# A chunked linear-attention and two-layer MLP kernel: the first group's order is rewritten (twelve idle transposes, output pieces back to back, one state decay on GpSimd, new orders of loads and weight halves)

## The reference, cut to what matters

```python
def _attn_ref(r, k, v, w, u):            # B, H, S, D = 4, 8, 768, 48
    for t in range(S):
        kt, vt, rt, wt = (k[:, :, t], v[:, :, t], r[:, :, t], w[:, :, t])
        cur = np.einsum('bhd,bhe->bhde', u[None] * kt, vt)
        y[:, :, t] = np.einsum('bhd,bhde->bhe', rt, state + cur)
        state = wt[:, :, :, None] * state + np.einsum('bhd,bhe->bhde', kt, vt)
# x: the 3072 tokens x 384 of y
h = x @ w_in                             # 384 -> 2048
g = np.where(h >= 1, h, np.where(h <= -1, 0.0, (h + 1) ** 2 / 4.0))
x = g @ w_out                            # 2048 -> 384
g = x @ w_gate                           # 384 -> 1536
out = ((g / (1 + np.exp(-g))) * (x @ w_val)) @ w_out2
```

## Time and profile before

| | |
|---|---|
| median of 3 runs | 984.63 us (984.63 to 985.52) |
| the profiled execution | 988.26 us, its span 986.4 us |
| PE busy | 961.5 us of the span (97%), mean granted clock 0.996 |
| DVE, ACT, POOL busy | 520.4, 404.3, 149.6 us |

### The profile page before, as it was taken

How to read it: one execution, slowest core, us unless ns; L and a number is a source line. 1 busy time by engine, 2 the same in 40 slices (tenths; PEclk the granted TensorE clock), 3 DMA queues, 4 the chain that set the end, 5 groups by cost and what they waited for, 6 DMA issues and landing times.

```text
span 986.4 us, 17455 instructions
## 1 busy us (share of the span) xinstructions
PE 961.5 (97%) x6874; PEld 942.9 (96%) x6874; DVE 520.4 (53%) x913; ACT 404.3 (41%) x849; POOL 149.6 (15%) x146
## 2 busy tenths in 40 slices
PE   5898999999999999999999999999999999999998
PEld 4788999999999999999999999999999999999997
DVE  7795757666566675675434443434334334434332
ACT  5755546445454554554575322222222222222222
POOL 6582120210202103020253400000000000000000
PEclk9998999999999999999999999999999999999999
DMA  8816131312212122200332201010100101010000
GB/s 244 275 44 165 58 96 44 96 56 74 83 57 80 61 86 58 82 26 1 113 105 85 85 1 49 1 49 1 49 0 0 48 0 48 0 48 0 24 1 26
DMA packets 23493, 59.52 MB, mean 60 GB/s; under 512 B 2689, under 2 KB 12033, under 8 KB 23425
## 3 DMA queue, kind: packets, MB, share of 16 engines
q1 hardware_dynamic: 23424, 58.59, 18.8%
HBM read 49.14 MB, written 9.44 MB: 59 GB/s over the span
## 4 chain that ended last, share of the span: by engine, by line
PE 91%; DVE 3%; DMA 2%; issue 1%; ACT 1%; SPq 0%; POOL 0%; DVEq 0%; ACTq 0%
PE bank L1168 48%; PE bank L1196 34%; PE bank L1222 3%; PE bank L1244 2%; PE bank L1239 2%; PE bank L1250 1%; PE bank L1214 1%; PE bank L1231 1%; DMA r_k_v_by_token<-in_rkv_token 1%; DMA ring<-in_w_gate 1%; DVE glo L1019 1%; DVE gate L1026 0%; DVE suf L929 0%; DVE state_decayed L980 0%; DMA ring<-in_w_out 0%
## 5 line engine op out<-in xcount | busy, mean ns | idle before, releaser
L770 ACT ACTIVATE ghi<-gate 128x384 fp32r<-128x384 f32 x224 | 117.2, 523 | 190.6 <-DVE gate L1038 95.4
L1019 DVE TENSOR_TENSOR glo<-gate,ghi 128x384 fp32r<-128x384 f32 x224 | 133.0, 594 | 114.8 <-ACT ghi L770 112.4
L1036 DVE TENSOR_TENSOR gate<-bank,gate 128x384 f32<-128x384 f32 x96 | 53.5, 558 | 215.0 <-ACT gate L889 215.0
L1168 PE MATMUL bank<-xhi,w2gv_ahi 128*128 128x384 f32 x480 | 161.3, 336 | 0.0
L1168 PE MATMUL bank<-xlo,w2gv_ahi 128*128 128x384 f32 x480 | 161.3, 336 | 0.0
L1168 PE MATMUL bank<-xhi,w2gv_alo 128*128 128x384 f32 x480 | 161.3, 336 | 0.0
L889 ACT ACTIVATE gate<-bank 128x384 f32<-128x384 f32 x96 | 47.2, 492 | 227.7 <-PE bank L1168 227.7
L1196 PE MATMUL bank<-ghi,w1ohi 128*128 128x384 f32 x384 | 134.5, 350 | 0.7 <-DVE glo L1019 0.7
L1168 PE MATMUL bank<-xhi,w1ihi 128*128 128x384 f32 x384 | 129.5, 337 | 5.0 <-DVE gate L1026 2.3
L1196 PE MATMUL bank<-glo,w1ohi 128*128 128x384 f32 x384 | 129.7, 338 | 0.0
L1196 PE MATMUL bank<-ghi,w1olo 128*128 128x384 f32 x384 | 129.6, 337 | 0.0
(11 more groups left out here) (93 smaller groups left out, 1532.0 us busy)
## 6 DMA issues: line engine op xcount, KB each, us to landing
r_k_v_by_token<-in_rkv_token SPq DMA_DIRECT2D x24, 576.0 KB, 5.3
k_r_by_channel<-in_kr_channel SPq DMA_DIRECT2D x24, 448.0 KB, 4.1
w_by_channel<-in_w_channel SPq DMA_DIRECT2D x24, 226.2 KB, 2.7
x_t<-ring SPq DMA_DIRECT2D x8, 576.0 KB, 3.0
x_raw<-x_t SPq DMA_DIRECT2D x8, 576.0 KB, 4.0
ring<-in_w_out SPq DMA_DIRECT2D x22, 192.0 KB, 3.4
out_t<-ring SPq DMA_DIRECT2D x7, 576.0 KB, 3.1
ring<-in_w_gate SPq DMA_DIRECT2D x12, 192.0 KB, 2.3
```

The costliest lines, as they stand in the source:

```text
L770: e.activation(ghi[j % 2][:, :], gate[j % 2][:, :], ACT.Copy).then_inc(M["hi", ph], 1)
L1019: e.tensor_tensor(glo[j % 2][:, :], gate[j % 2][:, :], ghi[j % 2][:, :].bitcast(F32), ALU.subtract)\
L1036: e.tensor_tensor(q, hid[j % 2][:, 0:T], q, ALU.mult).then_inc(M["t", 2], 1)
L1168: m = e.matmul(out, w_of(a, k), x_of(b_, k), start=start and i == 0, stop=stop and i == total - 1)
```

## The change

Only group 0 and what is prepared in it for the groups 1 and 2 is touched. Sizes, tiles and the arithmetic of each instruction stay.

- PE: twelve transposes of the identity into the bank of `KT(2)`, in front of the wait of `KT(2)` for its scaled input. In `FIRST_FILLS` the three `Y` come together, then the three `XT`, then `ST(2)`. Group 1's attention pieces come one slot later (4, 6, 7, 9, 10, 12, 13), and in slot 13 ACT and DVE drain `XT(2)` before their knee.
- The decay of the state for window 2 of group 0 is taken from ACT (8 instructions of 48x48) to POOL (2 of 48x192).
- `lo` halves: DVE keeps chunk 3 alone; POOL makes the other 31. `hi` halves on ACT: 8 in front of the `XT` drains, 9, then 11 behind the first two knees, and then by `HI_FIRST`.
- DVE in front of slot 0: drains of `Y`, then `XT`, then `ST(2)`; `w1_lo(3)`, `suffix_scan(1,0)`, the two knees, and only then `prefix_scan(1,0)` and `sum_w(0)`. Scans, scalings and sums of group 1 move by up to one slot; group 2's scans from slots 10, 13, 14 to 11, 14, 15. `w_beyond` has two halves, so that a check doesn't wait for the sum before.
- SP: the first 13 chunks all come right behind group 0's loads; group 1's loads are mixed with two sets of four chunks; the last chunks come before `load_w(2, w)`.

```diff
                ("KT", 2, 0), ("ST", 1, 0), ("AT", 2, 0), ("AT", 2, 1),
-               ("Y", 1, 0), ("XT", 0, 0), ("Y", 2, 0), ("XT", 1, 0), ("ST", 2, 0), ("XT", 2, 0)]
+               ("Y", 1, 0), ("Y", 2, 0), ("XT", 0, 0), ("XT", 1, 0), ("XT", 2, 0), ("ST", 2, 0)]
+WARM = 12
 NBANK = 3
...
 DIAG_SLOTS = {2: 0, 4: 1, 7: 2}
-WIN_SLOTS = {j: tuple(FILLS.index(f) for f in visit) for j, visit in zip((3, 5, 6, 8, 9, 11, 12), VISITS)}
+def visits_at(slots):
+    return {j: tuple(FILLS.index(f) for f in visit) for j, visit in zip(slots, VISITS)}
+WIN_SLOTS = visits_at((3, 5, 6, 8, 9, 11, 12))
+WIN_FIRST = visits_at((4, 6, 7, 9, 10, 12, 13))
+XT_FIRST = 13
...
-CHECK_FIRST = {0: 1, 2: 2}
-SCAN_FIRST = {1: 1, 4: 2}
-SCALE_FIRST = {0: 0, 2: 1, 7: 2}
-DIAG_FIRST = {2: 0, 4: 1, 6: 2}
-DVE_LO = 4
-LO_FIRST = {0: 7, 1: 11, 3: 15, 4: 19, 6: 23, 8: 27, 10: 31}
-PRODUCTS_AT = {8: 0, 13: 1, 20: 2}
-VALUES_AT = {12: 0, 18: 1, 25: 2}
+CHECK_FIRST = {0: 1, 3: 2}
+SCAN_FIRST = {1: 1, 5: 2}
+SCALE_FIRST = {0: 0, 2: 1, 8: 2}
+DIAG_FIRST = {2: 0, 5: 1, 7: 2}
+SCAN_SLOTS_FIRST = {11: 0, 14: 1, 15: 2}
+DVE_CHUNK = 3
+HI_FIRST = {0: 13, 1: 13, 2: 15, 3: 18, 4: 21, 5: 24, 6: 27, 7: 30, 8: 32}
+PRODUCTS_AT = {10: 0, 17: 1, 22: 2}
+VALUES_AT = {16: 0, 23: 1, 28: 2}
...
+def win_slots(g):
+    return WIN_FIRST if first(g) else WIN_SLOTS
+def scan_slots(g):
+    return SCAN_SLOTS_FIRST if first(g) else SCAN_SLOTS
...
         checked, _ = place("w_checked", [PR, NPAIR * WIN], mybir.dt.bfloat16)
-        beyond, _ = place("w_beyond", [PR, OPS_CHECK], F32)
+        beyond, _ = place("w_beyond", [PR, 2, OPS_CHECK + 2], F32)
         bad, _ = place("w_bad", [PR, OPS_CHECK + 1], F32)
...
         w1_at = at[0]
+        assert w1_at % 64 == 32
         w1i = [place(f"w1i{n}", [P, J1, KT * P], F32R)[0] for n in ("hi", "lo")]
...
-            if (c + 1) % DVE_LO == 0:
-                wait(wlo_d, (c + 1) // DVE_LO)
+            if c == DVE_CHUNK:
+                wait(wlo_d, 1)
             else:
-                wait(wlo, c + 1 - (c + 1) // DVE_LO)
+                wait(wlo, c + 1 if c < DVE_CHUNK else c)
...
             load_tok(0, 2)
-            load_w1(3)
-            for w in range(NW):
-                load_w(1, w)
-            load_w1(RING - 4)
-            for w in range(NW):
-                load_kr(1, w)
-                load_tok(1, w)
-            load_w1(14)
+            load_w1(RING - 1)
+            load_w(1, 0)
+            load_kr(1, 0)
+            load_w(1, 1)
+            load_tok(1, 0)
+            load_w1(4)
+            load_kr(1, 1)
+            load_w(1, 2)
+            load_tok(1, 1)
+            load_w1(4)
+            load_kr(1, 2)
+            load_tok(1, 2)
+            load_w1(2 * J1)
             for w in range(NW):
                 load_w(2, w)
-            load_w1(2 * J1)
...
             def w1_lo(c):
-                if (c + 1) % DVE_LO == 0:
+                if c == DVE_CHUNK:
                     return
...
+            def decay_second():
+                w = 2
+                e.wait_ge(scan, OPS_SCAN * w + 1)
+                e.wait_ge(st_out, 2 * w)
+                e.wait_ge(diag_p, NW * OPS_DIAG)
+                for i in range(2):
+                    r0, c0 = 64 * i, D * i
+                    rows = slice(r0, r0 + D)
+                    e.wait_ge(st_dec, OPS_DECAY * w + i * (OPS_DECAY // 2))
+                    wt = suf[rows, w, 0::SEG].rearrange("q (p o) -> q p o", o=1).to_broadcast([D, NPAIR, D])
+                    e.tensor_tensor(sbar[twin(0, w)][rows, :, c0:c0 + D], st[rows, :, :], wt, ALU.mult).then_inc(st_dec, OPS_DECAY // 2)
+                e.wait_ge(st_dec, OPS_DECAY * (w + 1))
...
             diag_products(0, 2)
-            w1_lo(0)
+            decay_second()
             diag_values(0, 1)
             diag_values(0, 2)
-            for c in range(1, 2 * J1):
+            for c in range(2 * J1):
                 w1_lo(c)
...
                 if w == 0:
-                    if first(g):
-                        e.wait_ge(tables, 1)
-                    else:
-                        e.wait_ge(w_sum, g + 1)
+                    e.wait_ge(tables, 1)
+                    if g > 1:
+                        e.wait_ge(w_sum, g)
                 e.wait_ge(ld["w", w], (g + 1) * 16)
...
                     e.activation(junk, src, ACT.Relu, bias=bias, scale=scale,
-                                 accum_out=beyond[:, m:m + 1]).then_inc(w_seen, 1)
+                                 accum_out=beyond[:, g % 2, m:m + 1]).then_inc(w_seen, 1)
...
             drain(0, fill_no(0, "KT", 2), 0)
-            more_hi(3)
-            decay_first(2)
-            more_hi(4)
+            more_hi(8)
             drain(0, fill_no(0, "XT", 0), 0)
-            more_hi(6)
             drain(0, fill_no(0, "XT", 1), 0)
-            more_hi(8)
             drain(0, fill_no(0, "XT", 2), 0)
+            more_hi(9)
             check_w(1, 0)
-            more_hi(11)
             knee(0, 0)
...
             knee(0, 1)
+            more_hi(11)
...
                     hi(2, 0, 0)
+                if first(g) and j == XT_FIRST:
+                    for f in win_slots(g)[j]:
+                        drain(g + 1, f, 1 - parity)
                 if not (last and j + 2 >= J1):
...
                     sig(0, j + 2 - J1)
-                if next_half:
-                    for f in WIN_SLOTS.get(j, ()):
+                if next_half and not (first(g) and j == XT_FIRST):
+                    for f in win_slots(g).get(j, ()):
                         drain(g + 1, f, 1 - parity)
                 if first(g):
-                    more_hi(done[0] + 2)
+                    more_hi(HI_FIRST.get(j, 2 * J1))
                     if j in CHECK_FIRST:
...
                 e.wait_ge(w_sum, g + 1)
-                e.tensor_tensor(bad[:, 0:OPS_CHECK], bad[:, 0:OPS_CHECK], beyond[:, :], ALU.add).then_inc(w_sum, 1)
+                e.tensor_tensor(bad[:, 0:OPS_CHECK], bad[:, 0:OPS_CHECK], beyond[:, g % 2, 0:OPS_CHECK], ALU.add).then_inc(w_sum, 1)
...
             diag_sum(0, 2)
-            sum_w(0)
-            drain(0, fill_no(0, "Y", 0), 0)
             drain_at(2)
-            drain(0, fill_no(0, "Y", 1), 0)
-            drain(0, fill_no(0, "XT", 0), 0)
-            drain(0, fill_no(0, "Y", 2), 0)
-            drain(0, fill_no(0, "XT", 1), 0)
-            drain(0, fill_no(0, "XT", 2), 0)
+            for kind in ("Y", "XT"):
+                for w in range(NW):
+                    drain(0, fill_no(0, kind, w), 0)
             drain(0, fill_no(0, "ST", 2), 0)
+            w1_lo(DVE_CHUNK)
             suffix_scan(1, 0)
-            w1_lo(3)
-            prefix_scan(1, 0)
             knee(0, 0)
...
             knee(0, 1)
+            prefix_scan(1, 0)
+            sum_w(0)
...
                     lo(2, 0, 0)
+                if first(g) and j == XT_FIRST:
+                    for f in win_slots(g)[j]:
+                        drain(g + 1, f, 1 - parity)
                 if not (last and j + 2 >= J1):
...
                         diag_sum(1, DIAG_FIRST[j])
-                    if j in LO_FIRST:
-                        w1_lo(LO_FIRST[j])
-                    if j == 5:
+                    if j == 6:
                         sum_w(1)
...
                         diag_sum(g + 1, DIAG_SLOTS[j])
-                if next_half:
-                    for f in WIN_SLOTS.get(j, ()):
+                if next_half and not (first(g) and j == XT_FIRST):
+                    for f in win_slots(g).get(j, ()):
                         drain(g + 1, f, 1 - parity)
                 if after_next:
-                    if j in SCAN_SLOTS:
-                        scan_window(g + 2, SCAN_SLOTS[j])
+                    if j in scan_slots(g):
+                        scan_window(g + 2, scan_slots(g)[j])
                 if after_next and j == SUM_SLOT:
...
                         e.wait_ge(ld["cst"], 16)
+                    for _ in range(WARM if first(g) and w == 2 else 0):
+                        e.transpose(out[:, 0:P], ident, ident)
                     e.wait_ge(scaled, 2 * (g * NW + w) + 1)
...
                 if next_half:
-                    for f in WIN_SLOTS.get(j, ()):
+                    for f in win_slots(g).get(j, ()):
                         do_fill(g + 1, f, 1 - parity)
```

More of the change, by code:

```diff
@@ L139, in build_program @@
         checked, _ = place("w_checked", [PR, NPAIR * WIN], mybir.dt.bfloat16)
-        beyond, _ = place("w_beyond", [PR, OPS_CHECK], F32)
+        beyond, _ = place("w_beyond", [PR, 2, OPS_CHECK + 2], F32)
         bad, _ = place("w_bad", [PR, OPS_CHECK + 1], F32)
-        ones, _ = place("ones", [PR, 1], F32)
+        ones, _ = place("ones", [PR, 9], F32)
+        ones = ones[:, 0:1]
         flag_at = (nc.sbuf_usable_end - 4) // 32 * 32
@@ L1043, in split_x @@
                                 ALU.subtract).then_inc(x2lo, 1)
-            e.memset(ones[:, :], 1.0)
+            e.memset(ones, 1.0)
             e.memset(bad[:, :], 0.0).then_inc(w_sum, 1)
```

(4 more changed lines are left out.)

## The result

| | before | after |
|---|---|---|
| median | 984.82 us (4 runs, 984.63 to 985.52) | 992.27 us (4 runs, 991.91 to 993.33) |
| profiled execution, its span | 988.26 us, 986.4 us | 992.52 us, 990.6 us |

The ratio is 1.0076, with a 95% interval of 1.0059 to 1.0094. The change made the kernel 7.5 us slower; forecast were 10.4 us less. The puzzle is that nearly every row that I had named as a test looks as forecast. The page first: span, and busy time, share and instructions of each engine.

What follows compares the result with a forecast made beforehand. PE's waits before 95 us bound what the change can give, its shift arriving undiminished. Gains 5.9 + 3.1 + 1.7 + 1.4 + 0.9 = 13.0 less 2.6 losses make 10.4: 974.2 us, range 970.5 to 979.0.

Steps and rivals of the forecast that it cites:

- POOL as the bound: Slower rival: POOL's lo halves hold PE up if each takes 2.5 us; 987 us, chance 0.02.
- The late chunk: Chunk 27 loaded before load_w(2,w): removes PE's 2.9 us wait near 82 us and 3.0 of half clock; gain 5.9.
- The transposes: Before KT(2), raise the clock at 22 to 23 us; 2.0 of the start's gain; no-earlier-rise rival 976.2 us, chance 0.14.
- the start: Up to tile_in(0,0): it starts at 29.0 us in place of 32.08; gain 3.1, or 1.1 without the earlier clock.
- the decay on POOL: Window 2's state decay as two POOL instructions, taken as 0.6 us each, from 22.75 to 23.9 us.
- The first knee: Prefix scan moved behind the knees: PE idle 0.6 us before tile_in(0,2) in place of 2.26; gain 1.7.
- POOL's wait: POOL no longer stands for diag_sum(1,0) with chunks 14 and on behind it; gain 1.4 us.
- for `glo`: DVE's fuller list up to lo(3) makes PE wait near 43 to 45 us; loss 1.0, bounds 0 and 3.9.
- the copy: Slot 15: scan_window(2,2) stands ahead of copy_out, which tile_out(1,0) wants; loss 1.3 us.
- DVE and POOL slowing each other: Rival: POOL's steady work stretches DVE's scans and scalings, loss 3.9 in place of 1.0; 978.2 us, chance 0.18.

Runs made afterwards that it cites:

- a1: The kernel before with only the new sizes of w_beyond and ones, moving the weights 64 bytes; 1001.02 us against 986.43, ratio 1.0147.
- d1: The kernel before with the loads of chunks 27 to 31 issued ahead of load_w(2,w); 981.66 us against 984.80, ratio 0.9972.
- a4: The kernel before with the twelve idle transposes alone, old addresses; 983.09 us against 986.43, ratio 0.9965.
- e2: The changed kernel at the old tile addresses, without the twelve transposes; 981.03 us, ratio to before 0.9943.
- e0: The changed kernel with its weights at the old addresses, a3 run once more; 977.40 us against 986.49, ratio 0.9910.
- a3: The changed kernel with the ones column kept inside w_bad, so the weights lie at the old address; 977.90 us against 986.43, ratio 0.9907.
- e3: The kernel before with the twelve transposes and chunks 27 to 31 loaded ahead of load_w(2,w); 979.84 us, ratio to before 0.9934.
- e1: e0 with copy_out moved ahead of slot 15's scan in group 0; 976.09 us, ratio to before 0.9896.

## Why the prediction was wrong

**The step that failed** is in the first paragraph: "what the change wins or loses is the shift of PE's work up to about 115 us, and it arrives at the end undiminished". The shift was there, 9.5 us in the profile. Behind it 4600 matmuls that the diff doesn't touch became 3.3 ns slower each, and the sum had no term for that: a1 has the new places alone and costs 14.6 us. The section on the change even says that sizes and tiles stay, which is wrong. The text of the diff shows half of the cause, `w_beyond` with two halves and an assertion on `w1_at % 64` (the nine columns of `ones` aren't in its shortened form); I costed it at nothing by never listing it. The assertion doesn't guard against the loss: with the weights at 57120 it holds, and the rate is the slow one. None of the rivals had this mechanism. The one on the slower side, POOL as the bound, didn't come: the last `lo` half of POOL ended at 77.9 us where 75 were forecast for a need at about 85.

**The late chunk, 5.9 us: the mechanism right, the size not.** The wait and the half clock went, but they were worth 3.1 us (d1). I took the length of the half-clock stretch from one execution, which I knew to be 3.6 us above the median, and took the sum off the median; and I counted on a full clock in every execution once the wait is gone, which d1 didn't have.

**The transposes.** Forecast were 2.0 us for the clock; measured are 3.3 (a4) and 3.6 (e2). The second is the cleaner measure: a4 keeps the wait near 82 us, and its executions go from 984.12 us at a mean clock of 0.996 to 981.92 at 1.000, while those of e0 and e2 lie within 0.8 us. The higher rate came even earlier than I put it: `KT(2)`, which took 0.98 us for four, takes 0.60 at 19.67 (0.79 in e0). In e2 the gain at `tile_in(0,0)` is 2.2 us, and the rest stands at the first knee and one `glo`. That this rest comes from a longer lead of ACT and DVE is argued and not shown, since a3 has these waits with the transposes.

**All else of the order.** Forecast 10.4 - 5.9 - 2.0 = 2.5 us, measured 2.4 (e3 to e0). Its parts: the start came out as worked out, and the decay on POOL took 1.16 us for two, as the 0.6 each that I took:

```profile
23.13 1.16 POOL L721 TENSOR_TENSOR state_decayed<-state,suf 48x192 f32<-48x192 f32 x2 [1.24 <-DVE state L1043]
```

The first knee left 0.5 us (forecast 0.6), POOL's wait went, 0.9 us appeared for `glo` (forecast 1.0) and 1.1 to 1.3 for the copy (forecast 1.3, e1 gives it back). By size the first group's whole gain was 3.1 + 3.3 + 2.4 = 8.8 us, measured 8.5 and 9.1 where I had 10.4. The 2.4 is itself the remainder between e3 and e0, so this sum tests the first two terms alone. That 8.8 comes near 10.4 is in part luck: the late chunk was 2.8 us too high and the transposes 1.3 too low. And that e1 gains just the 10.4 us of the forecast is chance, since it has a move that the forecast took as a loss.

**DVE and POOL slowing each other** did not decide. The mean of `lo` on DVE from 28 to 80 us:

```profile
L1055 DVE TENSOR_TENSOR glo<-gate,ghi 128x384 fp32r<-128x384 f32 x12 | 9.3, 774 | 3.1 <-ACT ghi L806 3.0
```

774 ns, as the 781 of the earlier trace rows; POOL's own became slower, at most 2.4 us against 1.9. But other two-input instructions of DVE in the window of 28 to 80 us did slow down: ```profile
L965 DVE TENSOR_TENSOR_SCAN suf<-w_by_channel,last_of_segment 112x516 f32<-112x516 f32 x3 | 5.2, 1731 | 0.0
...
L990 DVE TENSOR_TENSOR k_r_by_channel<-k_r_by_channel,w_by_channel 112x512 f32<-112x512 f32 x3 | 4.5, 1497 | 0.0
...
L987 DVE TENSOR_TENSOR k_r_by_channel<-k_r_by_channel,suf 112x512 f32<-112x512 f32 x3 | 3.1, 1036 | 0.0
```

In the same window of before they have 1343, 1227 and 737 ns, and e0 and e3, on one chip, show the same gap (1729, 1497, 1042 against 1344, 1226, 735). So this rival's mechanism may well have been at work, some 2.5 us of DVE's time with the prefix scan's 0.3 us of gain taken off, but PE's wait for `glo` stayed at 0.9 us. That POOL's steady work is the reason isn't tested by itself.

That GpSimd takes about twice as long for a two-input operation (Trainium skill, GPSIMD Engine Reference, 4.1) agrees with the trace, 1.01 us against 0.56 where each works undisturbed; it cost nothing because POOL had slack.

## What to carry to other kernels

Before a diff is costed by its instructions, work out which tiles its new sizes move, and treat a shifted matmul operand as a change to every matmul; afterwards compare the step from one matmul's start to the next in a stretch that the diff doesn't touch, since neither the busy share, nor the waits, nor the clock shows it. Pin the distance between moving and stationary tiles by placing small tiles behind them, and hold a new order at the old addresses when it is judged. A stall's price that is read in one execution slower than the median may be too high, as it was here (5.9 us against 3.1).

## What the runs showed of the hardware that was not expected

- The time from start to start in a stream of 128x384 matmuls with a weight load each changed with the distance in the partition between its moving and its stationary tiles: 173.3 ns at 40544, 40640 and 40704 bytes, 175.6 at 40576, 176.7 at 40608 and 40672 (phase 2). In this kernel it is worth 14.6 to 16 us of 980.
- In the slow layouts the granted clock is 1.00 and PE is busy 100%, and the step is 176.7 ns also where no other engine and no transfer is at work.
- The half-clock stretch behind a wait of 2.9 us had different lengths in profiled executions of kernels that had the same wait: over 6.4 us in before's, 3.4 us in a1's.
- Twelve transposes of a constant in a hole of 2.4 us brought the full rate by 19.67 us (`KT(2)` in 0.60 us; in e0 somewhat later, 0.79 us), where without them it came near 27 us.
- Without the long wait near 82 us the mean granted clock of d1's executions still went from 0.997 to 1.000, and their times from 983.85 to 980.62 us, mostly with it.
- The granted clock of a window doesn't show the slow level at the start. Before's window from 19.66 to 27.30 us reads 1.00 (PE busy, then clock, DMA share, GB/s), while its four `KT` matmuls take 0.98 us and its `Y` 1.90, against 0.60 and 1.09 after the change; only the durations tell:

```profile
19.66:27.30 7.64, 7.64 (x87) 1.00 0.65 196
```
